# A mixture-of-experts kernel: the third tile's down product ahead of the fourth's up product, GpSimd's weights behind the table, the places behind the sixth tile's x

## The chip, the cores and the metric

One core of a Trainium2 chip. The time is that of one execution of the whole program on the device, in microseconds (us). Before the change it is 1092.1 us, the median of three runs (1090.98 to 1092.83).

The engines are TensorE (PE in the profile; PEld is its weight load), VectorE (DVE), ScalarE (ACT), GpSimd (POOL) and SyncE (SP), which issues most transfers. Each works through its own list of instructions in order, and they wait for each other through semaphores.

## The reference

The program computes three things in a row: attention with a window of 64 keys, a gated feed-forward layer, and a layer of eight experts of which each token uses two. The change lies in the third. Its reference, cut to what matters:

```
logits = x @ w_gate
noisy_logits = logits + np.log1p(np.exp(x @ w_noise)) * noise
top2 = np.argpartition(-noisy_logits, 2, axis=1)[:, :2]
... top2_w: a softmax over the two
for e in range(E):                       # 8 experts
    for k in range(2):
        mask = top2[:, k] == e
        h = np.maximum(x[mask] @ w1[e], 0.0)          # 512 -> 1024
        out[mask] += top2_w[mask, k, None] * (h @ w2[e])   # 1024 -> 512
```

There are 2304 tokens of 512 numbers, so 4608 pairs of a token and an expert.

## The kernel before

The second layer works in six chunks of 384 tokens. Behind each chunk its 384 rows are scattered to DRAM (`routed_rows`), each row to two places, sorted by expert. The expert stage then takes 43 tiles of 128 sorted rows (`ETILES`), numbered t = 0 to 42 here and in the code; the third tile is t = 2. For each tile:

- SP loads the tile's rows (`load_rows`, four transfers of 64 KB) into one of two buffers `x_row`, when the tile two before has been turned. VectorE turns them (`dve_xT_turn`) into PSUM bank 6 and splits them in a high and a low part (`dve_xT`: `xT_high`, `xT_low`).
- TensorE multiplies by w1: `pe_up2`, 24 products of 128x512, in two halves of 12 in banks 0 and 1. "Up t" below. Each value is a high and a low part, and three products stand for one; these three are a triple.
- VectorE takes the relu out of PSUM (`dve_relu`, one operation for each half).
- TensorE transposes it: `pe_hT`, eight transposes in banks 2 and 3; "transposes t". VectorE splits them in `hT_high` and `hT_low` (`dve_hT`, a pair of operations for each half).
- TensorE multiplies by w2: `pe_down2`, 24 products in bank 5; "down t". The first 12 use the first half of `hT`, the others the second.
- VectorE copies the result out (`dve_y`, the tile `y_row`), and SP stores it to DRAM (`store_rows`, 256 KB). There is one `y_row`, so `dve_y` waits until the last store has landed.

The order of the work is written out by hand, engine by engine. In the steady order TensorE does transposes t - 1, up t, down t - 1, and VectorE does `hT` t - 1, relu t, x t + 1, y t - 1. Two buffers hold the weights of two experts; expert e's tiles use slot e % 2. Which slot, which expert and which row a tile takes is known only when all tokens are routed. It stands in a table in SBUF (`tab`), which VectorE reckons while tiles 0 to 2 run. These three use the first expert, which is the one with the most tokens in the first five chunks, so they need no table. The last part of the table is written by `dve_table_rows` (L1603 to L1609), which raises `table_done`; then SP can load tile 3's rows and TensorE can address tile 3's weights (`entry`, four `TENSOR_LOAD`s in a round).

GpSimd makes the low part of each weight (`expert_piece_low`, L683: two subtractions of 128x512 for each of 16 pieces of a pair of experts), behind ScalarE, which issues the loads of the raw weights (512 KB each) and makes the high part (L1274). Before the change GpSimd waits for `columns_done` (L1597, just ahead of the last part of the table) between piece 7 and piece 8 of the first pair: pieces 8 to 15 are the second expert's.

Two more parts of VectorE's work serve the end of the program, when the rows of `expert_rows` are gathered for each token: `dve_places` and `dve_combine`. They stand in tile 3's and tile 4's rounds.

## Time and profile before

| | us |
|---|---|
| median of three runs | 1092.1 |
| profiled execution | 1091.84 |
| its span | 1090.0 |
| TensorE busy in the span | 1066.4 |
| VectorE busy | 577.0 |
| GpSimd busy | 394.7 |
| ScalarE busy | 322.6 |

The profile is one execution. The span goes from its first to its last recorded work, and the rest of the execution's time lies around it. All times in rows count from the span's start. A row of the timeline gives the start, the time from there to the end of the group, the engine, the line, the operation with what it writes and reads, how many there are, and in brackets how long the engine idled before and what ended that. Matmuls overlap, so starts tell more than durations. The expert stage begins at 567 us.

### The profile page before, as it was taken

The numbers are of one execution on the slowest core, as the hardware profiler recorded it, in microseconds if no ns is written. First come the engines' busy times: TensorE is split into PE (matmuls) and PEld (weight loads), VectorE is DVE, ScalarE is ACT, GpSimd is POOL, SyncE is SP. The second block draws the span as 40 slices with busy tenths as digits, with TensorE's granted clock in tenths as the row PEclk, the third lists the DMA queues.
The fourth block names the chain that finished last, engine by engine and source line by source line (L and its number), as shares of the span: only waits on it lengthen the run. The fifth ranks groups of instructions, "written<-read, shape, count | busy, mean of one in ns | idle before, by whom it ended". The sixth has DMA issues, their size and how long they took to land.

```text
span 1090.0 us, 20075 instructions
## 1 busy us (share of the span) xinstructions
PE 1066.4 (98%) x6053; PEld 931.8 (85%) x6054; DVE 577.0 (53%) x1212; ACT 322.6 (30%) x710; POOL 394.7 (36%) x367
## 2 busy tenths in 40 slices
PE   8989999999999999999999999999999999999997
PEld 7778989999999999999987788888888888888886
DVE  6677335344353453453448765556556555555553
ACT  7996113143332432432452102030302011110222
POOL 4557992220220220220185407070605233150486
PEclk9999999999999999999999999999999999999999
DMA  7876434411411311211084526172525345232576
GB/s 223 262 239 211 146 115 171 139 58 19 127 59 30 115 58 29 96 59 29 20 249 153 159 49 202 39 202 49 174 63 142 102 102 148 75 100 51 159 227 236
DMA packets 199347, 133.18 MB, mean 122 GB/s; under 512 B 128720, under 2 KB 160864, under 8 KB 199296
## 3 DMA queue, kind: packets, MB, share of 16 engines
q1 hardware_dynamic: 177440, 75.14, 25.4%
q10 hardware_dynamic: 16032, 38.47, 10.7%
q0 software_dynamic: 5824, 18.95, 5.1%
q8 instruction: 24, 0.39, 0.2%
q14 instruction: 27, 0.22, 0.1%
HBM read 85.87 MB, written 42.73 MB: 118 GB/s over the span
## 4 chain that ended last, share of the span: by engine, by line
PE 89%; POOL 4%; DMA 2%; ACT 1%; DVE 1%; issue 1%; SPq 0%; DVEq 0%; ACTq 0%; POOLq 0%
PE bank L817 25%; PE bank L976 21%; PE bank L992 21%; PE bank L849 13%; PE bank L1005 3%; POOL mlp_weights L578 2%; PE bank L763 2%; PE bank L790 1%; DMA k_sb<-in_kT 1%; PE bank L773 1%; ACT p_sb L1127 1%; POOL mlp_weights L575 1%; PE bank L757 1%; DMA raw_mlp<-in_w_out 1%; PE bank L893 1%
## 5 line engine op out<-in xcount | busy, mean ns | idle before, releaser
L817 PE MATMUL bank<-x_parts,mlp_weights 128*128 128x384 f32 x1704 | 310.8, 337 | 2.0 <-POOL mlp_weights L578 2.0
L817 PEld LDWEIGHTS bank<-x_parts,mlp_weights 128*128 128x128 f32 x1704 | 298.2, 188 | 8.9 <-issue 2.4
L976 PE MATMUL bank<-expert_parts,xT_high 128*128 (+1 forms) x688 | 216.8, 396 | 1.7 <-DVE xT_low L1676 1.7
L992 PE MATMUL bank<-expert_parts,hT_high 128*128 (+1 forms) x688 | 212.3, 390 | 4.2 <-DVE hT_low L1687 4.2
L683 POOL TENSOR_TENSOR expert_parts<-raw_expert_a,expert_parts 128x512 fp32r<-128x512 f32 x64 | 81.3, 1303 | 239.3 <-ACT expert_parts L1274 239.0
L849 PE MATMUL bank<-mlp_weights,hidden_parts 128*128 128x512 f32 x648 | 162.1, 395 | 0.0
L992 PEld LDWEIGHTS bank<-expert_parts,hT_high 128*128 128x128 f32 x688 | 129.0, 188 | 31.8 <-POOL expert_parts L683 2.9
L976 PEld LDWEIGHTS bank<-expert_parts,xT_high 128*128 128x128 f32 x688 | 125.8, 188 | 26.2 <-issue 2.3
L849 PEld LDWEIGHTS bank<-mlp_weights,hidden_parts 128*128 128x128 f32 x648 | 120.3, 188 | 23.4 <-issue 1.0
L976 PE MATMUL bank<-expert_parts,xT_low 128*128 (+1 forms) x344 | 134.5, 391 | 0.0
L992 PE MATMUL bank<-expert_parts,hT_low 128*128 (+1 forms) x344 | 134.3, 390 | 0.0
L1430 DVE TENSOR_TENSOR hidden<-bank,sigmoid 128x384 f32<-128x384 f32 x72 | 40.1, 557 | 144.0 <-ACT sigmoid L1179 143.6
L1274 ACT CAST expert_parts<-raw_expert_a 128x1024 fp32r<-128x1024 f32 x32 | 33.5, 1049 | 270.0 <-PE bank L992 249.4
L1697 DVE TENSOR_SCALAR relu<-bank 128x512 f32<-128x512 f32 x86 | 59.0, 690 | 84.4 <-PE bank L976 84.4
L1704 DVE COPY y_row<-bank 128x512 f32<-128x512 f32 x43 | 29.7, 692 | 114.4 <-PE bank L992 111.7
L650 POOL DMA_INDIRECT routed_rows<-y_sb,slot_now x36 | 35.8, 995 | 145.4 <-DVE slot_now L1506 136.2
L1190 ACT CAST hidden_parts<-hidden 128x384 fp32r<-128x384 f32 x72 | 37.0, 513 | 157.1 <-DVE hidden L1433 150.4
L683 POOL TENSOR_TENSOR expert_parts<-raw_expert_b,expert_parts 128x512 fp32r<-128x512 f32 x64 | 81.0, 1296 | 2.4 <-ACT expert_parts L1274 2.4
L1179 ACT ACTIVATE sigmoid<-bank 128x384 f32<-128x384 f32 x72 | 35.4, 492 | 148.4 <-PE bank L817 148.2
L976 PEld LDWEIGHTS bank<-expert_parts,xT_low 128*128 128x128 f32 x344 | 64.6, 188 | 13.8
L992 PEld LDWEIGHTS bank<-expert_parts,hT_low 128*128 128x128 f32 x344 | 64.6, 188 | 13.3
L1436 DVE TENSOR_TENSOR hidden_parts<-hidden,hidden_parts 128x384 fp32r<-128x384 f32 x72 | 47.9, 665 | 46.2 <-ACT hidden_parts L1190 46.2
(207 smaller groups left out, 1200.5 us busy)
## 6 DMA issues: line engine op xcount, KB each, us to landing
raw_expert_a<-in_w ACTq DMA_DIRECT2D x32, 512.0 KB, 4.2
raw_expert_b<-in_w ACTq DMA_DIRECT2D x32, 512.0 KB, 4.5
x_row<-routed_rows SPq DMA_DIRECT2D x172, 64.0 KB, 2.5
expert_rows<-y_row SPq DMA_DIRECT2D x43, 256.0 KB, 2.0
expert_rows<-zeros SPq DMA_DIRECT2D x4, 2304.0 KB, 11.3
v_sb<-in_v SPq DMA_DIRECT2D x32, 256.0 KB, 3.7
q_sb<-in_qT SPq DMA_DIRECT2D x16, 288.0 KB, 3.7
k_sb<-in_kT SPq DMA_DIRECT2D x16, 288.0 KB, 4.1
```

The lines of the kernel that those rows point to most:

```text
L650: nc.gpsimd.indirect_dma_start(out=xs_dram, out_offset=bass.IndirectOffsetOnAxis(ap=slot_now[:, t, r:r + 1], axis=0), in_=y_sb[:, t, :], i ...
L683: nc.gpsimd.tensor_tensor(ew_sb[:, slot, 2 * kind + 1, at:at + 512], raw_exp(q)[:, half * 512:half * 512 + 512], ew_sb[:, slot, 2 * kind, ...
L817: last = nc.tensor.matmul(bank[:, 0:CHUNK], w_sb[:, i, wp, at:at + P], xp[:, par, part, k, :], start=n == 0, stop=n == 3 * KB - 1)
L849: last = nc.tensor.matmul(ps[3 + t][:, 0:D], hp[:, i % 2, part, t * P:(t + 1) * P], w_sb[:, i, wp, 2 * KB * P:COLS], start=i == 0 and n == ...
L976: last = nc.tensor.matmul(ps[half][:, 0:512], (xTh, xTl)[xp][:, buf, k, :], ew_sb[:, bass.ds(slot, 1), wp, k * F2 + half * 512:k * F2 + ha ...
L992: last = nc.tensor.matmul(ps[5][:, 0:D], (hTh, hTl)[hp][:, f, :], ew_sb[:, bass.ds(slot, 1), 2 + wp, f * D:(f + 1) * D].rearrange("p a n - ...
L1179: nc.scalar.activation(sig[:], ps[2 * i % 3][:, 0:CHUNK], ACT.Sigmoid).then_inc(sig_done, 1)
L1190: nc.scalar.copy(hp[:, i % 2, 0], h_sb[:]).then_inc(hh_done, 1)
L1274: nc.scalar.copy(ew_sb[:, slot, 2 * kind, piece * 1024:piece * 1024 + 1024], raw_exp(q)).then_inc(expert_high, 1)
L1430: nc.vector.tensor_tensor(h_sb[:], ps[2 * i % 3][:, 0:CHUNK], sig[:], ALU.mult).then_inc(gated, 1)
L1436: nc.vector.tensor_tensor(hp[:, i % 2, 1], h_sb[:], hp[:, i % 2, 0].bitcast(F32), ALU.subtract).then_inc(hl_done, 1)
L1697: nc.vector.tensor_scalar(relu[:, half * 512:half * 512 + 512], ps[half][:], 0.0, None, ALU.max).then_inc(relu_done, 1)
```

## The change

- TensorE: half of down 1, transposes 2, the other half, down 2, and only then up 3. Then the first half of up 4, transposes 3, the second half of up 4 and down 3. From tile 5 on the steady order holds. `pe_down2` can do one half; down 2 goes to bank 4. The first half of down 1 raises `second_tile_half_done`, which the first half of `hT` 2 waits for.
- VectorE: an order to match; `dve_places` moves from tile 3's round to tile 4's, behind the sixth tile's x (t = 5), and `dve_combine` from tile 4's to tile 5's.
- SP: tile 0's store goes out ahead of tile 3's rows, and each later store one place earlier in the list.
- GpSimd: piece 8 waits for `table_done` instead of `columns_done`.

```
# SP
             sp.wait_ge(table_done, 1)
             sp.wait_ge(scattered, 16 * ONE + 96 * CHUNKS)
+            store_rows(0)
             load_rows(3, 1)
             load_rows(4, 0)
-            store_rows(0)
+            store_rows(1)
             with sp.Fori(0, (ETILES - 5) // 2) as m:
                 for a in range(2):
                     load_rows(2 * m + (5 + a), (5 + a) % 2)
-                    store_rows(2 * m + (1 + a))
-            for t in range(ETILES - 4, ETILES):
+                    store_rows(2 * m + (2 + a))
+            for t in range(ETILES - 3, ETILES):
                 store_rows(t)
# GpSimd
             scatter(CHUNKS - 1)
-            pool.wait_ge(columns_done, 1)
+            pool.wait_ge(table_done, 1)
             for q in range(8, 16):
                 expert_piece_low(0, q)
# TensorE
+        def y_bank(t):
+            return ps[4] if isinstance(t, int) and t == 2 else ps[5]
+
+        def pe_down2(pe, t, slot, expert, halves=(0, 1)):
+            if halves[0] == 0:
+                pe.wait_ge(expert_low, 16 * expert + 16)
+                if not (isinstance(t, int) and t in (0, 2)):
+                    pe.wait_ge(y_row_done, ONE + t)
+            n = 3 * 4 * halves[0]
+            for half in halves:
+                pe.wait_ge(hTl_done, 2 * t + 1 + half)
+                for f in range(4 * half, 4 * half + 4):
...
+            last.then_inc(tile_done if halves[-1] == 1 else second_tile_half_done, 1)
...
             pe_up2(pe, 2, 0, 0, 0, (1,))
-            pe_down2(pe, 1, 0, 0)
+            pe_down2(pe, 1, 0, 0, (0,))
+            pe_hT(pe, 2)
+            pe_down2(pe, 1, 0, 0, (1,))
+            pe_down2(pe, 2, 0, 0)
             pe.wait_ge(table_done, 1)
...
-            tile(3, 1)
-            tile(4, 0)
+            fourth = entries(3)
+            pe_up2(pe, 3, 1, *fourth)
+            fifth = entries(4)
+            pe_up2(pe, 4, 0, *fifth, (0,))
+            pe_hT(pe, 3)
+            pe_up2(pe, 4, 0, *fifth, (1,))
+            pe_down2(pe, 3, *fourth)
# VectorE
+                if isinstance(t, int) and t == 2 and b == 0:
+                    dve.wait_ge(second_tile_half_done, 1)
...
             dve_hT(dve, 1)
             dve_relu(dve, 2)
+            dve_hT(dve, 2, (0,))
+            dve_y(dve, 1)
+            dve_hT(dve, 2, (1,))
             dve_xT(dve, 3, 1, 1)
-            dve_y(dve, 1)
-            for t, extra in ((3, dve_places), (4, dve_combine)):
+            dve_y(dve, 2)
+            dve_xT(dve, 4, 0, 2)
+            dve_relu(dve, 3)
+            for t, extra in ((4, dve_places), (5, dve_combine)):
                 dve_hT(dve, t - 1)
                 dve_relu(dve, t)
                 dve_xT(dve, t + 1, (t + 1) % 2, (t + 1) // 2)
...
             with dve.Fori(0, (ETILES - 7) // 2) as m:
-                tile(2 * m + 5, 0, m + 3)
                 tile(2 * m + 6, 1, m + 3)
-            tile(ETILES - 2, (ETILES - 1) % 2, (ETILES - 1) // 2)
+                tile(2 * m + 7, 0, m + 4)
```

VectorE's list from the last write of the table on. Before: `hT` 1, relu 2, x 3 and y 1.

```order
L1609 CAST tab<-tend 128x8
L1685 CAST hT_high<-bank 128x512
L1687 TENSOR_TENSOR hT_low<-bank,hT_high 128x512
L1685 CAST hT_high<-bank 128x512
L1687 TENSOR_TENSOR hT_low<-bank,hT_high 128x512
L1697 TENSOR_SCALAR relu<-bank 128x512 x2
L1666 STREAM_TRANSPOSE bank<-x_row 128x512
L1674 CAST xT_high<-bank 128x512
L1676 TENSOR_TENSOR xT_low<-bank,xT_high 128x512
L1704 COPY y_row<-bank 128x512
```

The same place in the changed kernel (L1706 and L1708 are `dve_hT`, L1718 relu, L1725 y, L1685 the turn).

```order
L1706 CAST hT_high<-bank 128x512
L1708 TENSOR_TENSOR hT_low<-bank,hT_high 128x512
L1718 TENSOR_SCALAR relu<-bank 128x512 x2
L1706 CAST hT_high<-bank 128x512
L1708 TENSOR_TENSOR hT_low<-bank,hT_high 128x512
L1725 COPY y_row<-bank 128x512
L1706 CAST hT_high<-bank 128x512
L1708 TENSOR_TENSOR hT_low<-bank,hT_high 128x512
L1685 STREAM_TRANSPOSE bank<-x_row 128x512
```

`hT` 2, in two halves around y 1, now stands ahead of x 3's turn.

TensorE's list at the end of down 1. Before: the last triple, the four reads of the table, transposes 2 and up 3.

```order
L992 MATMUL bank<-expert_parts,hT_high 128x512 x2
L992 MATMUL bank<-expert_parts,hT_low 128x512
L365 TENSOR_LOAD tab
...
L1005 MATMUL bank<-ident,relu 128x128 x8
L967 ISA
L976 ISA
L976 MATMUL bank<-expert_parts,xT_high 128x512
```

In the changed kernel, from the end of down 1's first half (L999 is the down product, L1012 the transposes, L978 the up product).

```order
L999 MATMUL bank<-expert_parts,hT_low 128x512
L1012 MATMUL bank<-ident,relu 128x128 x8
L999 MATMUL bank<-expert_parts,hT_high 128x512 x2
...
L366 TENSOR_LOAD tab
L366 ISA x2
L969 ISA
L978 ISA
L978 MATMUL bank<-expert_parts,xT_high 128x512
```

Behind transposes 2 stand twelve triples now (the rest of down 1 and the whole of down 2) ahead of up 3's first product, and two reads of the table instead of four.

SP's list around the wait for the table. Before: tile 3's rows, tile 4's rows, then the store of y 0.

```order
L365 TENSOR_LOAD tab [waits scattered,xT_done,table_done,ye_zeroed]
L365 ISA x2
L540 ISA
L540 DMA x_row<-routed_rows 32x16x32
...
L545 DMA expert_rows<-y_row 128x512 [waits y_row_done]
```

In the changed kernel (L541 are the rows, L546 the store).

```order
L546 DMA expert_rows<-y_row 128x512 [waits scattered,y_row_done,table_done,ye_zeroed]
L366 TENSOR_LOAD tab [waits xT_done]
L366 ISA x2
L541 ISA
L541 DMA x_row<-routed_rows 32x16x32
```

The store of y 0 has moved ahead of tile 3's four transfers, and carries the waits with it.

## Rows read from the trace of the kernel before

**Rows 1.** Windows: busy time and number of instructions by engine, clock, DMA.

```profile
594.40:628.50 34.10, 29.67 (x137) 24.10 (x136) 26.64 (x58) 5.14 (x5) 15.94 (x13) 1.00 0.59 163
628.50:1070.00 441.50, 441.50 (x2100) 368.77 (x2100) 251.99 (x385) 69.68 (x78) 161.60 (x137) 1.00 0.44 119
```

**Rows 2.** Timeline of TensorE, 560 to 630 us.

```profile
594.02 0.39 PE L976 MATMUL bank<-expert_parts,xT_low 128*128 128x512 f32 x1
596.87 0.70 PE L992 MATMUL bank<-expert_parts,hT_high 128*128 128x512 f32 x2 [2.46 <-DVE hT_low L1687]
...
602.43 1.04 PE L1005 MATMUL bank<-ident,relu 128*128 128x128 f32 x8
605.16 0.73 PE L976 MATMUL bank<-expert_parts,xT_high 128*128 x2 [1.69 <-DVE xT_low L1676]
...
616.17 1.03 PE L1005 MATMUL bank<-ident,relu 128*128 128x128 f32 x8
...
622.93 0.72 PE L992 MATMUL bank<-expert_parts,hT_high 128*128 x2 [0.28 <-DVE hT_low L1687]
...
628.55 1.06 PE L1005 MATMUL bank<-ident,relu 128*128 128x128 f32 x8
```

**Rows 3.** Timeline of TensorE, one round of the loop.

```profile
640.37 1.03 PE L1005 MATMUL bank<-ident,relu 128*128 128x128 f32 x8
641.16 0.71 PE L976 MATMUL bank<-expert_parts,xT_high 128*128 x2
...
646.69 0.61 PE L992 MATMUL bank<-expert_parts,hT_high 128*128 x2
...
652.14 1.04 PE L1005 MATMUL bank<-ident,relu 128*128 128x128 f32 x8
```

**Rows 4.** Timeline of VectorE, 560 to 642 us.

```profile
587.86 0.22 DVE L1583 TENSOR_SCALAR tiles_int<-tiles_int 128x8 int32<-128x8 int32 x1
...
591.83 1.12 DVE L1605 TENSOR_SCALAR tab<-tab 1x43 int32<-1x43 int32 x1
592.88 1.30 DVE L1607 TENSOR_SCALAR tab<-tend 128x8 int32<-128x8 f32 x1
594.21 1.19 DVE L1609 CAST tab<-tend 128x8 int32<-128x8 f32 x1
595.32 0.68 DVE L1685 CAST hT_high<-bank 128x512 fp32r<-128x512 f32 x1
...
597.96 1.28 DVE L1697 TENSOR_SCALAR relu<-bank 128x512 f32<-128x512 f32 x2
602.56 0.73 DVE L1666 STREAM_TRANSPOSE bank<-x_row 128x512 f32<-128x512 f32 x1 [3.32 <-DMA x_row<-routed_rows]
...
614.00 0.16 DVE L1514 TENSOR_SCALAR w_now<-w_now 128x3 f32<-128x3 f32 x1
...
620.63 0.69 DVE L1704 COPY y_row<-bank 128x512 f32<-128x512 f32 x1
```

**Rows 5.** Timeline of GpSimd, 555 to 680 us.

```profile
590.39 4.99 POOL L683 TENSOR_TENSOR expert_parts<-raw_expert_a,expert_parts 128x512 fp32r<-128x512 f32 x4 [0.27 <-DVE table_columns L1597]
...
653.55 5.06 POOL L683 TENSOR_TENSOR expert_parts<-raw_expert_a,expert_parts 128x512 fp32r<-128x512 f32 x4 [41.45 <-ACT expert_parts L1274]
```

**Rows 6.** The chain of work that ended last: start, us, what.

```profile
598.71 3.82 DMA x_row<-routed_rows
```

**Rows 7.** Line 540, 575 to 632 us: landing of tile rows.

```profile
DMA to landing us min/median/max: 2.2/2.7/5.8
```

**Rows 8.** Line 545, 575 to 632 us: landing of the stores.

```profile
DMA to landing us min/median/max: 2.0/3.2/5.6
```

**Rows 9.** Line 365, 623 to 629 us: TensorE's reads of the table.

```profile
L365 PEldq TENSOR_LOAD <-tab x4: 297/303/310, 625.4 to 627.6; - x4
```

**Rows 10.** Timeline of VectorE, one round of the loop.

```profile
647.50 0.72 DVE L1666 STREAM_TRANSPOSE bank<-x_row 128x512 f32<-128x512 f32 x1
...
652.44 0.69 DVE L1704 COPY y_row<-bank 128x512 f32<-128x512 f32 x1 [2.77 <-PE bank L992]
```

More of the change, by code:

```diff
@@ L333, in attention_moe_kernel @@
         tile_done = sem("tile_done")
+        second_tile_half_done = sem("second_tile_half_done")
         y_row_done = sem("y_row_done")
@@ L980, in pe_up2 @@
                 last.then_inc(up_done, 1)
-        def pe_down2(pe, t, slot, expert):
-            pe.wait_ge(expert_low, 16 * expert + 16)
-            if not (isinstance(t, int) and t == 0):
-                pe.wait_ge(y_row_done, ONE + t)
-            n = 0
-            for f in range(FB2):
-                if f % 4 == 0:
-                    pe.wait_ge(hTl_done, 2 * t + 1 + f // 4)
-                for wp, hp in PRODUCTS:
-                    last = nc.tensor.matmul(ps[5][:, 0:D], (hTh, hTl)[hp][:, f, :],
-                                            ew_sb[:, bass.ds(slot, 1), 2 + wp, f * D:(f + 1) * D].rearrange("p a n -> p (a n)"),
-                                            start=n == 0, stop=n == 3 * FB2 - 1)
-                    n += 1
-            last.then_inc(tile_done, 1)
+        def y_bank(t):
[9 more added lines that the diff above has]
+                for f in range(4 * half, 4 * half + 4):
+                    for wp, hp in PRODUCTS:
+                        last = nc.tensor.matmul(y_bank(t)[:, 0:D], (hTh, hTl)[hp][:, f, :],
+                                                ew_sb[:, bass.ds(slot, 1), 2 + wp, f * D:(f + 1) * D].rearrange("p a n -> p (a n)"),
+                                                start=n == 0, stop=n == 3 * FB2 - 1)
+                        n += 1
+            last.then_inc(tile_done if halves[-1] == 1 else second_tile_half_done, 1)
         def pe_hT(pe, t):
@@ L1030, in pe_experts, with entries @@
             pe_up2(pe, 2, 0, 0, 0, (1,))
-            pe_down2(pe, 1, 0, 0)
+            pe_down2(pe, 1, 0, 0, (0,))
+            pe_hT(pe, 2)
+            pe_down2(pe, 1, 0, 0, (1,))
+            pe_down2(pe, 2, 0, 0)
             pe.wait_ge(table_done, 1)
+            def entries(t):
+                return entry(pe, t + T_SLOT, 1), entry(pe, t + T_E, E - 1)
             def tile(t, buf):
-                now = entry(pe, t + T_SLOT, 1), entry(pe, t + T_E, E - 1)
-                before = entry(pe, t + (T_SLOT - 1), 1), entry(pe, t + (T_E - 1), E - 1)
+                now = entries(t)
+                before = entries(t - 1)
                 pe_hT(pe, t - 1)
@@ L1680, in dve_hT @@
                 dve.wait_ge(hT_done, 2 * t + b + 1)
-                if b == 0 and not (isinstance(t, int) and t == 0):
+                if isinstance(t, int) and t == 2 and b == 0:
+                    dve.wait_ge(second_tile_half_done, 1)
+                elif not (isinstance(t, int) and t == 0):
                     dve.wait_ge(tile_done, t)
@@ L1703, in dve_y @@
                 dve.wait_ge(y_row_out, 16 * ONE + 16 * t)
-            nc.vector.tensor_copy(y_row[:], ps[5][:, 0:D]).then_inc(y_row_done, 1)
+            nc.vector.tensor_copy(y_row[:], y_bank(t)[:, 0:D]).then_inc(y_row_done, 1)
         def dve_experts(dve):
```

## The prediction

> **What bounds the kernel now.** I read the busy time by stretch first. From 628.5 us to 1070 us TensorE is busy in all of 441.5 us; from 594.4 to 628.5 it is busy 29.67 of 34.10 us [rows 1]. So the long run of expert tiles is bound by TensorE, and idle time stands in the first tiles only. The granted clock is 1.00 in both stretches, the 2.4 GHz level, so no clock is there to be won.
>
> Then I read the timeline of TensorE in the bad stretch [rows 2]. The last triple of tile 2's up product starts at 594.02. Triples follow each other in 0.68 us, so the next product could start at about 594.25; it starts at 596.87, waiting for VectorE's `hT_low`. After the transposes at 602.43 tile 3's up product starts at 605.16, waiting for `xT_low`. Tile 2's down product starts at 622.93 with another wait for `hT_low`, and the transposes that open tile 5's round start at 628.55.
>
> For the undisturbed pace I take a round of the loop [rows 3]: transposes at 640.37, down at 646.69, the next transposes at 652.14. So transposes and up take 6.32, a down 5.45, a round 11.77 us. Split further: eight transposes take 0.79 (up starts at 641.16), an up or down of 24 products 5.45, and the first triple behind transposes costs 0.08 more (6.32 - 0.79 - 5.45).
>
> **What is in the stretch.** From 594.25 up to the transposes that open tile 5's round (628.55) both orders hold the same work: down 1, transposes 2, up 3, down 2, transposes 3, up 4 and down 3 [rows 2]. Undisturbed that is five products of 5.45, 27.25 us, two sets of transposes, 1.58, and 2 x 0.08: 28.99 us. It took 34.30. So at most 5.31 us can be won here, and nothing in the loop. They are 2.6 us ahead of down 1, 1.9 ahead of up 3 (605.16 against 602.43 + 0.79), 0.44 ahead of down 3 and 0.17 ahead of tile 5's transposes (below), and 0.2 of slower first triples behind the waits.
>
> **The wait for the table (GpSimd).** Three small VectorE operations that write the table take 1.12, 1.30 and 1.19 us and end at 592.95, 594.18 and 595.40; a like operation from SBUF to SBUF, on 128x8 integers, took 0.22 us at 587.86 [rows 4]. GpSimd runs four subtractions back to back from 590.39, 1.25 us each, which end at 591.64, 592.89, 594.14 and 595.38 [rows 5]. Each slow operation ends within 0.06 us of one of GpSimd's. I take them as held up by these, so the change, which lets GpSimd start only when the table is written, gives them 0.2 us each: the table is ready at 591.83 + 0.6 = 592.4 instead of 595.4, 3.0 us earlier. The bounds are 0 (they are slow by themselves) and 3.0.
>
> The Trainium skill (SBUF — State Buffer, "Who interferes with whom") says the same of the mechanism: a VectorE copy or tensor_scalar in a two-port mode needs the port pair that GpSimd also uses, and whoever comes second waits through the whole instruction. By that rule the 3.0 us are real and the first rival below nearly falls; the trace agrees, with the three ends above.
>
> What GpSimd loses: its sixteen subtractions begin at 592.4 instead of 590.39, 2.0 us later, and with them ScalarE's loads of raw weights. Before they were done at 612.1 (it then idles 41.45 us up to 653.55, when the first expert's last tile releases its slot) [rows 5]. They will be done at 614.1; the second expert starts after 652. Nothing waits.
>
> **The new order, step by step.** VectorE: `hT` of tile 1 starts at 592.4 in place of 595.32; its four operations and the next take 0.66 each (595.32 to 597.96) [rows 4]. The first half is in SBUF at 592.4 + 1.4 = 593.8; TensorE saw it 0.15 us later before (596.72 to 596.87), so it can start at 593.95, ahead of 594.25. The 2.6 us wait goes. Relu of tile 2 is done at 596.4.
> TensorE: half of down 1 to 596.97, transposes 2 (0.79) to 597.76, the rest of down 1 (2.80) to 600.56, down 2 to 606.01. The first half of `hT` 2 may be written once the half down 1 is over, 597.5 to 598.9: early. The second half stands behind y 1. In the loop y starts 0.30 after the next engine step (652.44 against 652.14) [rows 3, 10], so y 1 starts at 600.86, and with three operations of 0.66 and 0.15 the half is there at 603.0; TensorE asks for it at 600.56 + 2.73 = 603.29. Margin 0.3 us: the tightest place.
> Then `xT` 3. VectorE's turn of it starts at 602.85, if the rows are there. Before, 7.1 us passed from the table (595.40) to the landing at 602.53 [rows 4, 6]. Now SP first issues y 0's store, for which I put 0.6 us (the 3.3 us from 595.40 to the last issue at 598.71 held a read of the table and three issues, so at most 1.1 each): 592.4 + 0.6 + 7.1 = 600.1. From turn to TensorE's start it was 2.60 us (602.56 to 605.16) [rows 2, 4], so `xT` 3 is ready at 605.45, and up 3 starts at 606.01 without a wait. The 1.9 us wait goes as well, since down 2 fills it.
> y 2 starts at 606.3, if y 1's store has landed: issued at about 601.9, landing 2.0 to 5.6 later [rows 8], at worst 607.5. `xT` 4 then follows in 3.3 us, at 609.6 to 610.8; up 4 asks for it at 611.46. Covered in both cases. Up 4's first half to 614.2, transposes 3, second half to 617.8, down 3 to 623.2.
> **The places.** They take 6.63 us (614.00 to 620.63) and are followed by y and `hT` [rows 4]. Before they started 2.17 us ahead of the transposes of their round (616.17) and made TensorE wait, 622.93 against 616.17 + 6.32 = 622.49, 0.44 us. Moved behind tile 5's x, they start when relu, turn and two splits are over. In the loop the relu's end and turn's start stand at 647.50, 0.81 behind the down's start, and three operations later is 2.9 behind it; before, places started 3.28 behind down 2's start (610.72, from 616.17 - 5.45). So the round gains 0.38 and keeps about 0.06 of wait. The table loads of TensorE's queue (four, started from 625.4 to 627.6, each with some bookkeeping behind it, ahead of the transposes at 628.55 [rows 2, 9]) cost 0.17 more there, which I keep at 0.1. So 0.15 of the 5.31 us comes back one round later. The combining part moves one round on with them and keeps its place between x and y of its round, where it delayed nothing; in a round of the loop VectorE idles 2.77 us ahead of y alone [rows 10], about what it takes.
>
> **The sum.** 5.31 - 0.15 = 5.15 us. Everything behind (weights, gathers, the last stores) is released by tiles and moves along. The profiled execution took 1091.84 us, 1.84 around its span of 1090.0: 1086.7. It lies 0.26 under the median of 1092.1, so against the median I predict 1086.9 us, -0.47%.
>
> **Rivals.**
> *The table stays slow* (the three operations are slow by themselves). Then the wait until 596.87 stays, 2.6 us, and only `xT` 3 and the places gain: 1092.1 - 2.5 = 1089.6. For it: they all write the table. Against: all three ends agree with GpSimd's, to 0.06 us. 7%.
> *The store in front of tile 3's rows delays them.* The store of 256 KB now goes out ahead of the four loads on the same queue. The most I can read is that its whole landing time, 2.0 to 5.6 [rows 8], comes on top: 602.1 to 605.7, where VectorE's turn may start at 603.4 at the latest. That costs 0 to 2.3 us: about 1088.2. For it: x rows took up to 5.8 us beside ScalarE's loads [rows 7]. Against: between the issues and their landings most is latency, which overlaps. 10%.
> The Trainium skill (DMA: Bandwidth & Descriptors, "Queues, rings and completion order") has the rule for it: each DMA engine takes the descriptors of one issuing engine's ring in order. By it the store's transfer is ahead; at 0 to 2.3 us as above, and the trace of before has no store ahead of rows that were waited for.
> *A slower loop.* In the loop SP now issues the rows of tile t behind the store of tile t - 4, where they went behind that of t - 5. y of t - 4 is written at 652.44 + 0.69, the rows are issued and landed within 7.1 + 0.6 us, 661, or 664 with the slowest landing; their turn is at 647.50 + 2 x 11.77 = 671.0 [rows 3, 10]. From 7 us more on, each microsecond costs one in each of 36 rounds: 1 us is 1123. 2%.
>
> **Chances.** The forecast 76%, with its own range 1085.9 to 1087.7 (the runs of before spread by 1.85, a median by less); the table 7%; the store 10%; the slower loop 2%; small waits at the 0.3 us margins that add up to a microsecond or two 5%. The range of 8 in 10 takes in most of the store's case: 1085.5 to 1089.2. Below it lies nearly nothing, since only 5.31 us of idle time stands there. 0.2%, what this kernel's measurement can tell, is 2.2 us: the table's rival lies at its edge, and I give half of it to each side. Faster is 93%, the same 5%, slower 2%.
>
> **What would show it.** The three table operations at about 0.2 us and no overlap with GpSimd's subtractions; TensorE's first down triple at 594.2 to 594.4; up 3 at 606.0 behind down 2 with no wait; tile 5's transposes at 623.2 to 623.4, then rounds of 11.77 as before. Operations of over a microsecond in the table with GpSimd idle would prove the first rival, a wait of VectorE's turn for `x_row` behind 603.4 the second, and any wait for `x_row` in the loop the third.

## The result, and the profile after

| | before | changed |
|---|---|---|
| first comparison, medians of 6 runs each | 1091.53 us | 1084.39 us |
| ratio | | 0.9936 (0.9924 to 0.9948): 7.0 us (5.7 to 8.3) |
| profiled run | 1091.84 us | 1084.60 us |
| its span | 1090.0 us | 1082.8 us |

Predicted were 1086.9 us, a range of 1085.5 to 1089.2, and a gain of 5.15. The sign and the three waits came out; the gain is larger, and the time lies below the range. Five of the runs below took 1.4 to 5.6 times as long as the others; they are left out of all times and ratios.

TensorE's waits of the changed kernel from 570 us to the end (us in total, times, longest):

```profile
PE bank L999 <- DVE hT_low L1708: 1.4, 1, 1.4
```

That one is ahead of the last down product, at 1071 us, and before had it too. The three waits of [rows 2] are gone. The stretch and the round behind it (columns as [rows 1]):

```profile
584.71:620.54 35.83, 35.83 (x174) 29.60 (x173) 24.75 (x65) 5.16 (x5) 22.18 (x19) 1.00 0.62 177
620.54:632.63 12.09, 12.09 (x57) 9.77 (x56) 11.33 (x27) 0.00 (x0) 0.00 (x0) 1.00 0.20 45
```

TensorE is busy in all of both. Its timeline (columns as [rows 2]), from down 1 to tile 5's transposes:

```profile
591.51 0.62 PE L999 MATMUL bank<-expert_parts,hT_high 128*128 128x512 f32 x2
...
594.24 1.04 PE L1012 MATMUL bank<-ident,relu 128*128 128x128 f32 x8
...
603.32 0.61 PE L978 MATMUL bank<-expert_parts,xT_high 128*128 x2
...
611.48 1.03 PE L1012 MATMUL bank<-ident,relu 128*128 128x128 f32 x8
...
620.54 1.04 PE L1012 MATMUL bank<-ident,relu 128*128 128x128 f32 x8
...
632.63 1.03 PE L1012 MATMUL bank<-ident,relu 128*128 128x128 f32 x8
```

This execution came to transposes 1 at 584.71, that of before at 587.45, though the code up to there is the same. So 2.74 us are added for the comparison with the prediction: first down triple 594.25 (forecast 594.2 to 594.4), up 3 at 606.06 (606.0), tile 5's transposes at 623.28 (623.2 to 623.4). VectorE at the table and at x 3 (against [rows 4]), and GpSimd (against [rows 5]):

```profile
589.09 0.17 DVE L1624 TENSOR_SCALAR tab<-tab 1x43 int32<-1x43 int32 x1
589.19 0.15 DVE L1626 TENSOR_SCALAR tab<-tend 128x8 int32<-128x8 f32 x1
589.38 0.17 DVE L1628 CAST tab<-tend 128x8 int32<-128x8 f32 x1
589.46 0.69 DVE L1706 CAST hT_high<-bank 128x512 fp32r<-128x512 f32 x1
...
600.00 0.72 DVE L1685 STREAM_TRANSPOSE bank<-x_row 128x512 f32<-128x512 f32 x1
...
603.78 0.69 DVE L1725 COPY y_row<-bank 128x512 f32<-128x512 f32 x1 [1.54 <-DMA expert_rows<-y_row]
```

```profile
589.64 5.03 POOL L685 TENSOR_TENSOR expert_parts<-raw_expert_a,expert_parts 128x512 fp32r<-128x512 f32 x4 [2.25 <-DVE tab L1628]
...
645.82 5.07 POOL L685 TENSOR_TENSOR expert_parts<-raw_expert_a,expert_parts 128x512 fp32r<-128x512 f32 x4 [34.34 <-ACT expert_parts L1293]
```

The three writes of the table take 0.17, 0.15 and 0.17 us in place of 1.12, 1.30 and 1.19. The turn of x 3 waits for nothing, y 2 waits 1.54 us for the store and nobody waits for y 2. GpSimd still idles 34 us.

So the stretch did what the prediction said. Most of what it did not say lies in the kernel before.

### The profile page after: what moved, and what is told of

The parts are those of the page before. It is cut to its first block, busy times and chain, and to the rows that moved or that the text cites. A ratio compares the mean times of both kernels' runs of the same rounds, so it can differ in the third digit from the quotient of the medians.

```text
span 1082.8 us, 20088 instructions
## 1 busy us (share of the span) xinstructions
PE 1067.5 (99%) x6053; PEld 933.3 (86%) x6054; DVE 573.6 (53%) x1212; ACT 322.6 (30%) x710; POOL 395.2 (37%) x367
## 4 chain that ended last, share of the span: by engine, by line
PE 92%; POOL 2%; DMA 1%; ACT 1%; issue 1%; another core or an unknown queue 1%; DVE 1%; POOLq 0%; DVEq 0%; ACTq 0%; SPq 0%
PE bank L819 27%; PE bank L978 20%; PE bank L999 19%; PE bank L851 14%; PE bank L1012 3%; PE bank L765 3%; PE bank L792 2%; PE bank L775 1%; PE bank L759 1%; DMA token_rows_b<-expert_rows,slots_u 1%; ACT p_sb L1146 1%; PE bank L895 1%; POOL token_rows_a L703 0%; DMA mask_sb<-in_c_mask 0%
## 5 line engine op out<-in xcount | busy, mean ns | idle before, releaser
L978 PE MATMUL bank<-expert_parts,xT_high 128*128 (+1 forms) x688 | 216.5, 396 | 0.0
L999 PE MATMUL bank<-expert_parts,hT_high 128*128 (+1 forms) x688 | 212.1, 390 | 1.4 <-DVE hT_low L1708 1.4
L999 PEld LDWEIGHTS bank<-expert_parts,hT_high 128*128 128x128 f32 x688 | 129.0, 188 | 28.7 <-issue 2.0
L978 PEld LDWEIGHTS bank<-expert_parts,xT_high 128*128 128x128 f32 x688 | 125.7, 188 | 24.4 <-issue 0.4
L978 PE MATMUL bank<-expert_parts,xT_low 128*128 (+1 forms) x344 | 134.3, 391 | 0.0
L999 PE MATMUL bank<-expert_parts,hT_low 128*128 (+1 forms) x344 | 134.1, 390 | 0.0
L1718 DVE TENSOR_SCALAR relu<-bank 128x512 f32<-128x512 f32 x86 | 58.9, 690 | 74.9 <-PE bank L978 74.9
L1725 DVE COPY y_row<-bank 128x512 f32<-128x512 f32 x43 | 29.7, 692 | 121.5 <-PE bank L999 105.3
L978 PEld LDWEIGHTS bank<-expert_parts,xT_low 128*128 128x128 f32 x344 | 64.5, 188 | 14.0
L999 PEld LDWEIGHTS bank<-expert_parts,hT_low 128*128 128x128 f32 x344 | 64.6, 188 | 13.4
L636 POOL TENSOR_TENSOR squares<-x_chunk 128x384 f32<-128x384 f32 x5 | 4.4, 887 | 186.6 <-DMA x_chunk<-xT_scratch 186.6
```

Source lines behind the costliest of these rows:

```text
L978: last = nc.tensor.matmul(ps[half][:, 0:512], (xTh, xTl)[xp][:, buf, k, :], ew_sb[:, bass.ds(slot, 1), wp, k * F2 + half * 512:k * F2 + ha ...
L999: last = nc.tensor.matmul(y_bank(t)[:, 0:D], (hTh, hTl)[hp][:, f, :], ew_sb[:, bass.ds(slot, 1), 2 + wp, f * D:(f + 1) * D].rearrange("p a ...
L1718: nc.vector.tensor_scalar(relu[:, half * 512:half * 512 + 512], ps[half][:], 0.0, None, ALU.max).then_inc(relu_done, 1)
```

## The experiments

"Stretch" below is the time from transposes 1 to transposes 4, in a kernel's one profile; "rest" is the span without it. Where a run is said to have a half clock, its mean granted clock is 0.998 or lower; 3.41 us at half clock in a span of 1090 us make 0.0016. This tells it nearly, not surely: every profile also ends at half clock, behind TensorE's last product, for 0.8 to 3.8 us, which make up to 0.0017. The profile of gpsimd_wait_alone (below) has 0.998 by this end alone (columns as [rows 1]):

```profile
580.00:640.00 60.00, 56.58 (x270) 46.37 (x269) 46.81 (x118) 6.21 (x6) 25.92 (x22) 1.00 0.49 143
1084.80:1088.50 3.70, 0.00 (x0) 0.00 (x0) 0.76 (x2) 0.00 (x0) 0.00 (x0) 0.50 0.58 223
```

The other eight profiles with 0.998 or less have a half clock in the stretch, and the eleven with more have none. No profile has two; a mean of 0.997 can be two, or one and a long end.

The runs stand in four groups, on three chips (the first group on one, the second on another, the last two on the third). In them the medians of the kernel before, beside which the others ran, were 1091.4, 1090.4, 1089.7 and 1090.3 us. So kernels are compared by their ratio to the runs of before beside them; the intervals of these ratios are 2 to 3.6 us wide.

**Both kernels again (before_again, after_again).**

> The kernel before, unchanged, timed against itself; nothing is left out. Its profile tells when the expert stage begins, which is what separates the theories on the 2.7 us that the changed kernel was ahead there. Chance theory (the attention stage waits for its loads a little more or less in each execution): the time is within 1.0 us of the kernel before, and the transposes of tile 1 begin anywhere from 584.7 to 588 us (before: 587.45, changed kernel 584.71), with TensorE's waits for loads and weights ahead of 570 us between 8 and 13 us. Rival (something of the changed program makes the earlier stages shorter): the transposes of tile 1 begin at 587.0 to 587.9 us again.

> The changed kernel again; nothing is left out. Stage theory (all of the lasting gain is in the first expert tiles): 4.4 to 5.4 us faster than the kernel before, and from tile 1's transposes to the transposes that open tile 5's round pass 35.8 us (before: 41.1 us). Rival (earlier stages are shorter too, lastingly): 6.5 to 8 us faster, and tile 1's transposes begin at 584.3 to 585.2 us again.

Measured: 1090.88 and 1084.04 us; the latter is 0.9930 of before (0.9917 to 0.9943). That is 7.6 us faster, beyond the 4.4 to 5.4 of the stage theory and in the range of its rival, though the profiles speak against the rival: the changed kernel's stretch is 35.83 us again, and it reached transposes 1 at 583.68. Before reached them at 583.50, 4 us earlier than in its first profile and earlier than either theory had it, so the 2.74 us were chance. But its stretch took 42.46 us in place of 41.10. Its TensorE timeline:

```profile
598.49 1.04 PE L1005 MATMUL bank<-ident,relu 128*128 128x128 f32 x8
601.31 0.72 PE L976 MATMUL bank<-expert_parts,xT_high 128*128 x2 [1.78 <-DVE xT_low L1676]
...
603.05 1.05 PE L976 MATMUL bank<-expert_parts,xT_high 128*128 x2
...
604.34 1.05 PE L976 MATMUL bank<-expert_parts,xT_high 128*128 x2
...
605.62 0.75 PE L976 MATMUL bank<-expert_parts,xT_high 128*128 x2
```

and the window of the slow triples (the 1.00 of the other rows is 0.50 here, the 1.2 GHz level):

```profile
602.60:605.90 3.30, 3.30 (x9) 2.59 (x8) 2.57 (x4) 1.05 (x1) 3.30 (x4) 0.50 1.01 270
```

Triples of 1.29 us in place of 0.68, behind the wait: up 3 takes 12.65 us up to transposes 3 where it took 11.01 in [rows 2]. From this comes the half-clock theory: TensorE's waits bring a half clock that the first profile did not happen to show.

**One part alone and undone (gpsimd_wait_alone, after_gpsimd_undone).**

```
# gpsimd_wait_alone: the kernel before with
-            pool.wait_ge(columns_done, 1)
+            pool.wait_ge(table_done, 1)
# after_gpsimd_undone: the changed kernel with
-            pool.wait_ge(table_done, 1)
+            pool.wait_ge(columns_done, 1)
```

> The kernel before with one line changed: GpSimd's piece 8 waits for the table and no longer for its columns. Nothing is left out. Port theory (the three table writes were held up by GpSimd's subtractions): they take 0.15 to 0.25 us each, the 2.6 us wait ahead of down 1 goes, tile 3's rows land 3 us earlier and the wait ahead of up 3 shrinks by 0.3: 2.9 us faster (2.4 to 3.3). Rival (the writes are slow by themselves): they still take over 1 us each, and the time is the same within 0.5 us.

> The changed kernel with GpSimd's wait put back to the table's columns; the order of TensorE, VectorE and SyncE stays new. Nothing is left out. Port theory: the table writes take 1.1 to 1.3 us each again, the wait ahead of down 1 is back with 2.6 us, and the new order alone is worth 2.5 us against the kernel before (2.0 to 3.0). Rival (the order alone gives it all, the table's time does not matter): 4.5 us or more faster.

Measured: alone 1089.93 us, ratio 0.9986 (0.9976 to 0.9996), 1.5 us faster where 2.9 were expected. Undone 1087.52 us, 0.9958 (0.9943 to 0.9974): 3.5 us slower than the changed kernel, but 4.6 us (2.8 to 6.2) faster than before where 2.5 were expected, so the surplus over the forecast is there without GpSimd's part too. The table's writes did as the port theory says: 0.17, 0.15 and 0.17 us alone, and 1.11, 1.31 and 1.19 undone, with the wait of 2.46 us back ahead of down 1. Alone, that wait is gone, but down 3 waits 1.76 us. VectorE's timeline at the places, and GpSimd beside it:

```profile
609.72 0.69 DVE L1514 TENSOR_SCALAR w_now<-w_now 128x3 f32<-128x3 f32 x1
610.45 0.18 DVE L1515 RECIPROCAL w_now<-w_now 128x3 f32<-128x3 f32 x1
610.66 1.00 DVE L1516 TENSOR_TENSOR w_now<-w_now 128x3 f32<-128x3 f32 x1
...
612.13 0.20 DVE L1617 TENSOR_REDUCE in_last<-of_last 128x6 f32<-128x48 f32 x1
612.37 0.54 DVE L1618 TENSOR_SCALAR needs<-in_last 128x6 int32<-128x6 f32 x1
```

```profile
607.83 5.06 POOL L683 TENSOR_TENSOR expert_parts<-raw_expert_b,expert_parts 128x512 fp32r<-128x512 f32 x4
```

The three operations of 0.69, 1.00 and 0.54 us take 0.16, 0.17 and 0.17 in the changed kernel, and they end here at 610.41, 611.66 and 612.91, each within 0.05 us of the end of one of GpSimd's subtractions. So the places lost 1.7 us to GpSimd's later subtractions. The Trainium skill (SBUF — State Buffer, "Who interferes with whom") counts an operation with two SBUF inputs among those that GpSimd's reads hold up, and a reduction as never held up: the 1.00 us beside 0.17 and the 0.20 us of the reduction, which is 0.20 in the changed kernel as well, agree. In this order the later start of GpSimd needs the later places.

**Products that nothing reads in the waits.** If the half clock comes from the idling, filling the waits takes it away, with nothing ready any earlier.

```
# filler_in_waits: the kernel before with
+        def filler(n):
+            for _ in range(n):
+                nc.tensor.matmul(ps[4][:, 0:512], ew_sb[:, 0, 0, 0:P], ew_sb[:, 0, 0, 0:512], start=True, stop=True)
+            filler(10)                       # ahead of down 1
             pe_down2(pe, 1, 0, 0)
...
                 pe_hT(pe, t - 1)
+                filler(fill)                 # 7 ahead of up 3
# filler_gpsimd_and_places: gpsimd_and_places (below) with filler(8) ahead of up 3
# filler_gpsimd_undone: after_gpsimd_undone with filler(10) ahead of the first half of down 1
```

> The kernel before with products that nothing reads put into TensorE's two longest waits: ten of 128x512 (0.23 us each, 2.3 us) ahead of down 1, which waited 2.46 us, and seven (1.6 us) ahead of up 3, which waited 1.7 us; they go to bank 4. Nothing becomes ready earlier. Half-clock theory (in most runs of the kernel before, TensorE's granted clock falls to 0.5 for 3.4 us once or twice behind these waits, and each such stretch costs 1.7 us; the one profile I predicted from had none): the mean granted clock of nearly all runs is 0.999 or 1.000 in place of 0.997 to 0.998, and the median falls by 1.5 to 2.5 us against before, to about 1089.5. Rival, that the half clock has nothing to do with the idling, or that the variable cost of before is elsewhere: mean clock 0.997 to 0.998 as before and the median within 0.7 us of it, or up to 0.3 us later by what the products stand over the waits.

> The kernel before with GpSimd's wait for the table and the places one round later, and eight products of 128x512 that nothing reads (1.8 us) in the one wait that is left there, 2.0 us for tile 3's x ahead of up 3. Without them half of that kernel's runs had a mean clock of 0.998 (mean 1087.4 us) and half 0.999 or 1.000 (1085.8 to 1087.6 us), and in its profile the half clock lay in up 3, behind the wait, where no later wait takes it up. Half-clock theory: mean clock 0.999 or 1.000 in all runs but one at most, and the median 0.5 to 1.5 us below the same kernel without the products: 3.7 to 4.7 us faster than before. Rival, that the clock follows something else, or that its fall costs nothing because something absorbs it: 0.998 in half of the runs, or 0.999 with the time of the kernel without the products, 3.3 us faster than before.

> The changed kernel with GpSimd's old wait (columns_done), and ten products that nothing reads in the wait of 2.46 us that this brings back ahead of down 1. Half-clock theory: mean clock 0.999 or 1.000 in all runs but one at most, and about 0.8 us faster than the same kernel without them (1.7 us in half of its runs), so 4.8 us faster than before and 2.4 to 2.8 us slower than the changed kernel. Rival: no change against the kernel without the products, 4.0 us faster than before.

Timeline of TensorE with the filler (L1010) ahead of down 1:

```profile
590.30 2.43 PE L1010 MATMUL bank<-expert_parts 128*128 128x512 f32 x10
```

The clock, over all kernels of the study:

| kernel | TensorE's waits in the stretch of the profiles, us | runs without a half clock (mean clock 0.999 or 1.000) |
|---|---|---|
| before, all groups | 2.46 and 0.4 to 1.8 | 14 of 93 |
| store_first_alone | 2.46, 1.9 | 0 of 12 |
| places_alone | 1.2, 2.8 | 2 of 12 |
| gpsimd_wait_alone | 1.7, 1.8 | 2 of 11 |
| x3_early | 2.46 | 5 of 9 |
| after_gpsimd_undone | 2.46 | 4 of 6 |
| gpsimd_and_places, twice | 2.0; 1.7 | 6 of 13 |
| all_but_order, twice | 1.2; 1.35 | 12 of 14 |
| the three with filler | 0.2 to 1.2; none; 0.2 | 11 of 12; 5 of 6; 7 of 7 |
| changed, and rows_first | none | 21 of 21 |

So the first half of the theory is shown: the same work and the same releases, only filled, went from 14 of 93 to 11 of 12. Its price on the whole time is not shown as clearly. filler_in_waits gave 1089.91 us, ratio 0.9993 (0.9984 to 1.0002), 0.8 us faster (0.2 slower to 1.7 faster) where 1.5 to 2.5 were expected and the rival said 0.7 at most; filler_gpsimd_and_places 1086.26 us, 0.9955 (0.9938 to 0.9971), 4.9 us faster (3.2 to 6.8), just above the 3.7 to 4.7 of its theory and with the rival's 3.3 in its interval; filler_gpsimd_undone 1086.22 us, 0.9961 (0.9947 to 0.9975), where the kernel without filler had 0.9958 on another chip: 0.8 us more or nothing more can't be told apart.

The profiles tell it better. Transposes 1 and 2 of after_gpsimd_undone, with the half clock, and of the same kernel with filler, without:

```profile
584.67 1.03 PE L1012 MATMUL bank<-ident,relu 128*128 128x128 f32 x8
598.31 1.04 PE L1012 MATMUL bank<-ident,relu 128*128 128x128 f32 x8
```

```profile
584.82 1.03 PE L1012 MATMUL bank<-ident,relu 128*128 128x128 f32 x8
597.11 1.04 PE L1012 MATMUL bank<-ident,relu 128*128 128x128 f32 x8
```

That is 13.64 against 12.29 us, and no later wait takes the 1.35 us up: the stretches are 39.94 and 38.59. The times of runs agree: over 218 runs of all kernels, a run at 0.998 takes 1.1 us (plus or minus 0.4) longer than one of the same kernel and group at 0.999 or 1.000, and one at 0.997 or less another 0.6 (plus or minus 0.5); one figure for each step is 0.87 (plus or minus 0.28). The half clock at the end is not what costs, since runs at 0.999 and at 1.000 differ by 0.05 us (plus or minus 0.5). But a run in which rows land late has a longer wait and may get the half clock with it, so a part of the 0.87 us can be the wait's. A third profile of before shows why it is less than 1.7:

```profile
595.91 1.01 PE L992 MATMUL bank<-expert_parts,hT_high 128*128 128x512 f32 x2
...
597.14 1.05 PE L992 MATMUL bank<-expert_parts,hT_high 128*128 128x512 f32 x2
...
602.33 1.04 PE L1005 MATMUL bank<-ident,relu 128*128 128x128 f32 x8
603.78 0.73 PE L976 MATMUL bank<-expert_parts,xT_high 128*128 x2 [0.42 <-DVE xT_low L1676]
```

Here the half clock fell in down 1. Transposes 2 came 1.6 us late (16.61 behind transposes 1, 14.98 in the first profile), and the wait for x 3 was 0.42 in place of 1.69: the wait took it up.

**The other parts (places_alone, gpsimd_and_places, store_first_alone, all_but_order, rows_first).**

```
# places_alone, gpsimd_and_places, all_but_order: the kernel before with
-            for t, extra in ((3, dve_places), (4, dve_combine)):
+            for t, extra in ((3, None), (4, dve_places), (5, dve_combine)):
# gpsimd_and_places, all_but_order: table_done for columns_done as well
# store_first_alone, all_but_order: SP's part of the change as well
# rows_first: the changed kernel with
-            store_rows(0)
             load_rows(3, 1)
+            store_rows(0)
             load_rows(4, 0)
```

> The kernel before with only the places and the combining part one round later. By the prediction's step the wait of 0.28 us ahead of down 3 goes and 0.15 us comes back a round later: 0.1 to 0.4 us faster than before. Collision theory says the same here, since GpSimd's subtractions start early and end before the places. Rival: the places' wait was larger in most runs than in the profile, 1 us or more faster.

> The kernel before with two parts of the change: GpSimd waits for table_done, and the places and the combining part stand one round later. TensorE's, SP's and the rest of VectorE's order are the old ones. Collision theory (GpSimd's later start gained only 1.4 us alone because its subtractions then lay over the places, which took 8.35 us in place of 6.63 and held up down 3 by 1.8 us): no wait ahead of down 3, the wait of 1.7 us ahead of up 3 stays, 1.5 to 2.1 us faster than with GpSimd's wait alone, so 3.0 to 3.6 us faster than before, about 1088.2. Rival, that the two are independent (as the prediction had it): 1.4 us plus 0.3 us, so about 1.7 us faster than before, 1089.8.

> The kernel before with SP's part of the change alone: y 0's store ahead of tile 3's rows, each later store one place earlier. In the old order y 1 waited 2.3 to 4.1 us for y 0's store; hT 2, relu 3, x 4 and the places follow y 1 on VectorE, and the places held up down 3 by 0 to 1.2 us. Theory that this spread is a part of what the prediction missed: y 1 starts right behind x 3, no wait ahead of down 2 or down 3, 0.3 to 1.0 us gained there, less 0.6 us for tile 3's rows, issued later: 0.4 us slower to 0.6 us faster than before. Rival (the store in front delays tile 3's rows by its whole landing): the wait ahead of up 3 grows by 2 us or more, and the kernel is 1 us or more slower than before.

> The kernel before with every part of the change but the new order of TensorE and VectorE: GpSimd's wait, the places one round later, and the stores one place earlier on SP. What is left to the order is the wait of 2.0 us for tile 3's x ahead of up 3 with its half clock. Expected: within 0.7 us of GpSimd's wait and the places alone (3.3 us faster than before), since y 1 no longer waits for y 0's store but nobody waited for y 1 there, while tile 3's rows are issued 0.6 us later: if anything 0.3 to 0.6 us slower. The new order is then worth about 3 us. Rival, that the store's landing was a cost of its own in most runs: 1 us or more faster than GpSimd's wait and the places alone.

> The changed kernel with tile 3's four row transfers issued ahead of y 0's store, in place of behind it; all else as changed. By the prediction's main case the store in front costs nothing, since tile 3's x is wanted only behind down 2: within 0.5 us of the changed kernel, about 1084.2; x row 3 lands 0.6 us earlier or more. y 1 waits for y 0's store, which is now issued 1.7 us later, but it is wanted only at half of down 1: if it lands late, TensorE waits ahead of down 2 and the kernel is 0.5 to 3 us slower. Rival, the store in front delays tile 3's rows: 0.5 to 2.3 us faster than the changed kernel.

| kernel | median | ratio, interval | faster than before by |
|---|---|---|---|
| places_alone | 1089.50 | 0.9991 (0.9981 to 1.0001) | 1.0 us |
| gpsimd_and_places | 1087.12 | 0.9963 (0.9948 to 0.9978) | 4.0 us |
| store_first_alone | 1089.76 | 0.9992 (0.9981 to 1.0003) | 0.9 us |
| all_but_order | 1085.68 | 0.9961 (0.9947 to 0.9975) | 4.2 us |
| rows_first | 1084.30 | 0.9940 (0.9925 to 0.9955) | 6.5 us |

rows_first is the changed kernel's time (within 0.5 us was expected): y 0's store in front neither costs nor brings anything that can be told. That rival is out, by the rows too: from the table's last write to the turn of x 3 it took 7.16 to 8.26 us in ten profiles with SP's old order, and 7.03, 7.18 and 7.38 in three with the store in front (VectorE waited for the rows in all of them). store_first_alone behaves alike: y 1 no longer waits, TensorE still waits 2.46 and 1.91 us. gpsimd_and_places gained 4.0 us (2.4 to 5.7) where the collision theory said 3.0 to 3.6 and the rival 1.7; run again it gave 2.7 us (1.5 to 3.9, below). The times lean to the theory, and the profiles decide it: neither has the wait ahead of down 3 that gpsimd_wait_alone had. places_alone (0.1 to 0.4 expected, 1 or more by its rival) can't be told from nothing, nor from either. all_but_order lies within 0.7 us of gpsimd_and_places, as expected.

**x 3's wait, and the order's worth (x3_early, changed_third, all_but_order_second, gpsimd_and_places_second), on one chip.**

```
# x3_early: the kernel before with
+            load_rows(3, 1, row_of=2)        # ahead of the wait for the table; tile 2's rows
             sp.wait_ge(table_done, 1)
-            load_rows(3, 1)
```

> The kernel before, but tile 3's rows are read from tile 2's place, ahead of the table, so that VectorE can turn them without waiting (tile 3 then works on the wrong rows; all the work is still done). Everything else waits as before: 2.46 us ahead of down 1 stays. The prediction's term for this wait was 1.9 us, from the one profile. If that was its size: 1.5 to 2.0 us faster than before. If the half clock and the later landings of other runs belong to it, as I now think: 2.3 to 3.2 us faster, no wait ahead of up 3, and a mean clock of 0.998 at the lowest in most runs, since only the wait ahead of down 1 is left.

> The changed kernel once more, beside the two kernels below on one chip. 6.5 to 7.5 us faster than before, mean clock 0.999 or 1.000 in all runs, 35.8 us from transposes 1 to transposes 4.

> The kernel before with every part of the change but TensorE's and VectorE's order. Its first profile had one wait, 1.2 us ahead of up 3, and 37.28 us from transposes 1 to transposes 4, 1.45 us more than the changed kernel. If that holds in most runs: 1.3 to 2.2 us slower than the changed kernel. If the first run was a lucky one and the wait is commonly 2.0 us with its half clock: 2.5 to 3.3 us slower.

> The same without SP's part. Its first profile had a wait of 2.0 us ahead of up 3 and 39.63 us in the stretch. If the store in front of tile 3's rows helps (y 1 no longer waits, and the landing was not later): 0.5 to 1.5 us slower than all but the order. If it does nothing: within 0.5 us of it.

| kernel | median | ratio, interval | stretch |
|---|---|---|---|
| before | 1090.25 | | |
| x3_early | 1088.27 | 0.9979 (0.9969 to 0.9989) | 40.41 |
| gpsimd_and_places_second | 1087.21 | 0.9975 (0.9964 to 0.9986) | 37.74 |
| all_but_order_second | 1086.48 | 0.9965 (0.9952 to 0.9978) | 37.45 |
| changed_third | 1084.21 | 0.9945 (0.9932 to 0.9958) | 35.83 |

The wait for x 3 is worth 2.3 us (1.2 to 3.4), at the edge between both theories. changed_third is 6.0 us faster than before (4.6 to 7.4) where 6.5 to 7.5 were expected. The order of TensorE and VectorE is worth 2.3 us here (1086.48 to 1084.21) on top of all other parts, between the two forecasts; the stretch gives 1.6 of them. The 0.7 us between the two kernels without it can't be told from nothing. What is left of the wait in all_but_order_second:

```profile
599.68 0.73 PE L977 MATMUL bank<-expert_parts,xT_high 128*128 x2 [1.35 <-DVE xT_low L1677]
```

**Two more profiles of before.**

> The kernel before, unchanged, for its profile. If the profile that I predicted from had a short stretch and slow stages ahead of it: 42 to 44 us from transposes 1 to transposes 4, a half clock of 3.4 us in the stretch, and 1045 to 1047 us in the rest of the span. Rival, that 41.1 us and 1048.9 us are common: 41 us again, and the missing 1.9 us of the gain are elsewhere.

> As before_third: 42 to 44 us in the stretch and 1045 to 1047 us in the rest if the first profile was lucky there, 41 us and 1049 us if it was common.

| | stretch | rest | half clock in the stretch |
|---|---|---|---|
| before, first profile | 41.10 | 1048.9 | none |
| before_again | 42.46 | 1046.5 | in up 3 |
| before_third | 41.09 | 1047.1 | in down 1 |
| before_fourth | 41.62 | 1046.3 | in down 1 |
| changed: after, after_again, changed_third, rows_first | 35.83, 35.83, 35.83, 35.84 | 1047.0, 1045.9, 1046.6, 1046.7 | none |

Half of this was expected: the rest was slow in the first profile and each new one has a half clock. That the stretch would then take 42 to 44 us was wrong, since both fell in down 1.

What makes the four stretches differ can be read off the rows, against the first profile. Tile 3's rows were turned 7.16 us behind the table's last write there, and 7.25, 7.50 and 8.01 in the others: 0.09, 0.34 and 0.85 us more. Down 3 waited 0.28 us there and not in the others: 0.38, 0.36 and 0.32 us less in that round. And the half clock in up 3 cost 1.64 us in before_again, those in down 1 nothing. The sums are 42.45, 41.08 and 41.63 us; measured were 42.46, 41.09 and 41.62.

## Why the prediction was right, and where it was wrong

The 1084.4 us of the first comparison lie below the range of 1085.5 to 1089.2. The step that failed is the clock, put at nothing; the base and the size of one wait add to the miss.

**The three waits (right).** The table's writes were held up by GpSimd, the wait ahead of down 1 is gone, down 2 fills the wait for x 3, and the three starts that were forecast came within 0.1 us. GpSimd's later start cost the changed kernel nothing. The first rival, a slow table, is out by the rows of 0.15 to 0.17 us, the second by rows_first, and the third by the loop: TensorE's only wait from 570 us on is that ahead of the last down.

**"So 0.15 of the 5.31 us comes back one round later" (too small).** The round from tile 5's transposes takes 12.09 us (12.08 to 12.14 in four profiles), where it took 11.82 or 11.83 in all four profiles of before: 0.27 us.

**"So no clock is there to be won" (the step that failed).** It was read from one execution's window at 1.00 [rows 1]. Three of the four profiles of before have 3.41 us at 0.50 in the stretch, and so have, by the mean clock, 79 of 93 runs; the changed kernel has none in 21. What it costs is an estimate: 1.0 us, if each of 93 runs counts one step at 0.998 and two at 0.997 or less (1.13 steps a run), at 0.87 us each. Measured directly, the filled waits gave 0.8 us (0.2 slower to 1.7 faster). The idle time of a profile does not show this. With it fails "below it lies nearly nothing, since only 5.31 us of idle time stands there", and the lower end of the range.

**"1.9 ahead of up 3" (too small).** The first profile had the shortest time from the table's last write to tile 3's turn of the ten with SP's old order, 7.16 us against 7.73 on average in the other nine. A wait ahead of up 3 is longer by as much, where no half clock ahead of it takes it up. In the changed kernel down 2 covers the later landings as well.

**The base (luck, or the chip).** The prediction took its 5.15 us from 1092.1 us, three runs. The 93 runs have a median of 1090.4 us, 21 runs in the changed order (five of them rows_first) 1084.2. The gain is 6.2 us by medians and 6.4 by means, and the interval of the first comparison holds both. The miss of 2.7 us against 1084.2 is thus 1.7 us of base and 1.0 us of gain. The base depends on the chip too: 34 runs of before on one chip have a median of 1091.2 us, the 59 others on the other two 1090.2, while the changed kernel took 1084.0 to 1084.3 on all three. Which chip the first comparison ran on is not on record.

**What the 6.4 us are.** In the four profiles of before the stretch takes 41.57 us on average, in the changed kernel 35.83; less the 0.27 us, 5.5 us. That much is shown. These four had 0.75 steps of half clock a run and the 93 had 1.13: by the estimate above 0.3 us more, of which later landings may be a part. The other 0.6 us stay open. They are no larger than the chance of the rest: 1047.2 us on average in these four and 1046.5 in the changed ones, but 1046.6 in fourteen profiles in TensorE's old order and 1046.5 in six in the new.

**The parts are not independent (not seen).** The prediction priced the places at 0.38 us by their start alone, and costed GpSimd's later start at nothing because the second expert is far away. It did not ask which VectorE operations the moved subtractions would come to lie beside. In the old order they are the places, at 1.7 us. In the change this cancelled, because the places moved too.

No kernel of the study beat the changed one.

## What to carry to other kernels

A wait of TensorE can cost more than its idle time: look in several profiles, or at the mean clock of every run, for a half clock behind it, and put a range's end where that would lead. The half clock costs its full time only where no later wait takes it up. A wait for a transfer is as long as that execution's landing: read its size from several profiles too. When work on one engine is moved because it held up another, list what it will lie beside in the new place.

## What the runs showed of the hardware

Two waits between dense products within a stretch of 41 us, at least one of them of 1.7 to 2.8 us, came with a half clock (a mean clock of 0.998 or less) in 110 of 128 runs, one wait of 1.7 to 2.5 us in 13 of 28, one of 1.2 to 1.35 us in 2 of 14, and none in 0 of 21. It was 3.41 us long in each of the eight profiles that have one. It began with the first product behind the wait (x3_early, at 594.27) or 1.2 us later (before_again, where TensorE started again at 601.31 and slowed at about 602.5). It was not there in each execution of the same program, and ten products of 0.24 us into a free bank kept it away, in 7 of 7 runs in place of 4 of 6 and, with seven more ahead of up 3, in 11 of 12 in place of 14 of 93. VectorE's operations of 0.15 to 0.20 us, from SBUF to SBUF, took 0.5 to 1.3 us beside GpSimd's subtractions and ended with one of them; one that started as a subtraction ended took 0.15 us (places_alone, at 589.10).
